# Keeping x by chunks and fetching the first expert's first 128 rows one step earlier, in a fused attention and expert kernel

## What is computed

```python
for t in range(S):                                   # attention
    cur = np.einsum('bhd,bhe->bhde', u[None] * kt, vt)
    y[:, :, t] = np.einsum('bhd,bhde->bhe', rt, state + cur)
    state = w[None, :, :, None] * state + np.einsum('bhd,bhe->bhde', kt, vt)
do_compute = x @ w_skip > 0                          # experts
e_idx = np.argmax(xc @ w_gate, axis=1)
for e in range(E):
    h = np.maximum(xc[mask] @ w1[e], 0.0)
    y[mask] = gate_w[mask, None] * (h @ w2[e])
out[do_compute] = xc + y
h = x @ w_in                                         # dense layer
g = h * np.clip(h + 3.0, 0.0, 6.0) / 6.0
return g @ w_out
```

## Time and profile before

| what | value |
|---|---|
| median of 3 runs | 697.08 us |
| time of the profiled execution | 699.52 us |
| its span in the profile | 697.7 us |
| granted TensorE clock, mean | 0.998 |
| PE, PEld, DVE, ACT, POOL busy | 98, 89, 55, 46, 20 % |
| attention / seam and experts / dense layer | about 0 to 141, 141 to 292, 293 to 697.7 us |

### The profile page before, as it was taken

One profiled execution on the slowest core, in us unless ns is written; L12 is line 12 of the kernel. 1 busy time (PEld: TensorE's weight loads), 2 busy tenths in 40 slices (PEclk: granted clock), 3 DMA queues, 4 the chain that ended last, 5 costly groups with the idle time before them and its releaser, 6 DMA issues.

```text
span 697.7 us, 13712 instructions
## 1 busy us (share of the span) xinstructions
PE 686.7 (98%) x5072; PEld 623.7 (89%) x5072; DVE 381.7 (55%) x788; ACT 323.8 (46%) x704; POOL 141.2 (20%) x190
## 2 busy tenths in 40 slices
PE   7999999999999999999999999999999999999998
PEld 5888888879999999899999999999999989998997
DVE  5677667678777777666543443343434333434333
ACT  5777777735555555554433333233333333324222
POOL 8757966543232321100000000000000000000000
PEclk9999999999999999999999999999999999999999
DMA  7888876718666668320023004000500050001001
GB/s 137 186 201 198 186 170 153 238 39 294 232 216 211 223 208 279 104 25 1 1 60 32 1 1 84 7 1 0 92 1 0 1 91 1 0 1 47 0 1 45
DMA packets 135161, 65.70 MB, mean 94 GB/s; under 512 B 110724, under 2 KB 130696, under 8 KB 135104
## 3 DMA queue, kind: packets, MB, share of 16 engines
q1 hardware_dynamic: 131088, 60.13, 33.6%
q0 software_dynamic: 2560, 4.60, 2.1%
q10 hardware_dynamic: 1456, 0.20, 0.2%
HBM read 53.37 MB, written 12.48 MB: 94 GB/s over the span
## 4 chain that ended last, share of the span: by engine, by line
PE 94%; DVE 2%; POOL 1%; issue 1%; DMA 1%; ACT 0%; another core or an unknown queue 0%; DVEq 0%; ACTq 0%; POOLq 0%
PE bank_A L1038 8%; PE bank_A L1039 8%; PE bank_A L1037 8%; PE bank_L L1037 4%; PE bank_L L1039 4%; PE bank_L L1038 4%; PE bank_P L1039 4%; PE bank_P L1038 4%; PE bank_P L1037 4%; PE bank_kT L1038 4%; PE bank_kT L1039 4%; PE bank_kT L1037 4%; PE bank_A L954 4%; PE bank_YT L1039 3%; PE bank_YT L1038 3%; PE bank_YT L979 3%
## 5 line engine op out<-in xcount | busy, mean ns | idle before, releaser
L1595 DVE TENSOR_TENSOR g_lo<-g,g_hi 128x512 fp32r<-128x512 f32 x96 | 66.5, 692 | 67.1 <-ACT g_hi L824 67.1
L824 ACT ACTIVATE g_hi<-g 128x512 fp32r<-128x512 f32 x96 | 60.7, 632 | 73.1 <-DVE g L1593 73.1
L1593 DVE SCALAR_TENSOR_TENSOR g<-cut,bank_A 128x512 f32<-128x512 f32 x60 | 41.2, 687 | 76.4 <-ACT cut L821 76.4
L821 ACT ACTIVATE cut<-bank_A 128x512 f32<-128x512 f32 x60 | 35.8, 597 | 94.2 <-PE bank_A L1039 93.7
L1039 PE MATMUL bank_A<-mT_hi,wi_lo 128*128 128x512 f32 x180 | 71.0, 394 | 0.0
L1038 PE MATMUL bank_A<-mT_lo,wi_hi 128*128 128x512 f32 x180 | 70.9, 394 | 0.0
L1037 PE MATMUL bank_A<-mT_hi,wi_hi 128*128 128x512 f32 x180 | 70.0, 389 | 0.0
L658 ACT ACTIVATE bank_A<-ident,own 128x128 f32<-128x128 f32 x188 | 58.1, 355 | 23.7 <-DVE A_sb L1293 18.7
L1593 DVE SCALAR_TENSOR_TENSOR g<-cut,bank_kT 128x512 f32<-128x512 f32 x36 | 24.7, 687 | 67.5 <-ACT cut L821 67.5
L821 ACT ACTIVATE cut<-bank_kT 128x512 f32<-128x512 f32 x36 | 21.5, 597 | 70.5 <-PE bank_kT L1039 70.5
L1037 PE MATMUL bank_kT<-mT_hi,wi_hi 128*128 128x512 f32 x108 | 42.1, 389 | 0.9 <-DVE mT_lo L1586 0.9
(11 more groups left out here) (333 smaller groups left out, 1807.1 us busy)
## 6 DMA issues: line engine op xcount, KB each, us to landing
raw<-in_moe_w_dram SPq DMA_DIRECT2D x24, 512.0 KB
raw<-in_moe_w_dram SPq DMA_DIRECT2D x7, 1536.0 KB
r_in<-in_r_dram SPq DMA_DIRECT2D x24, 192.0 KB, 3.6
v_in<-in_v_dram SPq DMA_DIRECT2D x24, 192.0 KB, 4.2
x_scratch<-y_sb SPq DMA_DIRECT2D x24, 192.0 KB, 2.3
k_in<-in_k_dram SPq DMA_DIRECT2D x23, 192.0 KB, 3.8
m_in<-x_scratch SPq DMA_DIRECT2D x20, 192.0 KB, 5.5
out_dram<-o_sb SPq DMA_DIRECT2D x10, 384.0 KB, 2.8
```

Of the source, the lines that this page charges most:

```text
L821: eng.activation(cut[f % 2][:, :], p_H[f % 3][:, :], ACT.Relu, bias=0.5, scale=1.0 / 6.0).then_inc(s_cut, 1)
L824: eng.activation(g_hi[f % 4][:, :], g[f % 2][:, :], ACT.Copy).then_inc(s_ghi, 1)
L1593: eng.scalar_tensor_tensor(g[f % 2][:, :], cut[f % 2][:, :], 1.0, p_H[f % 3][:, :], ALU.min, ALU.mult).then_inc(s_g, 1)
L1595: eng.tensor_tensor(g_lo[f % 4][:, :], g[f % 2][:, :], g_hi[f % 4][:, :].bitcast(F32), ALU.subtract).then_inc(s_glo, 1)
```

## The change

1. x is stored by chunks: row s of chunk c and batch b lies at (c*4 + b)*128 + s. The rows' numbers (`identify`, `own_rows`), the dense layer's blocks (now one chunk of all four batches) and the places of its output rows follow.
2. The first tile's part 0 now holds tokens of chunks 0 to 4 less one, that is 0 to 3. `skip` is worked out one chunk earlier (at b = 1 of chunk 5, for the carry of chunk 4, instead of at b = 2).
3. SP reads the two columns of `listed` by two DMAs: column 0 when chunks 0 to 3 have landed, after the store of (1, 5); column 1 when chunk 4 has landed, between the stores of (2, 5) and (3, 5).
4. POOL gathers part 0 ahead of the scatters of chunk 4, and waits for both columns before the scatters of group 5.
5. PE transposes part 0 right after the last step and puts the two column parts of the first pass around the count of group 6. There are 2 + 2 + 5 + 4 + 8 = 21 `go_on` transposes instead of 5 + 9 + 9 + 8 = 31.
6. ACT's `rows_high(0, 0)` comes ahead of `rows_out(3, 5)`. DVE waits for both columns where it waited for one DMA, and does `rows_low(0, 0)` ahead of `route_slot` of group 6.

```diff
-ON = (8,)
+ON = (2, 5, 4, 8)
         def x_rows(b, c):
-            return x_dram[b * S + c * P:b * S + (c + 1) * P, :]
+            return x_dram[(c * B + b) * P:(c * B + b + 1) * P, :]
@@ SP
-            store(B - 2, NC - 1)
-            for i, done in enumerate(s_slots):
-                eng.wait_ge(done, 16 * B * len(range(i, NC - 1, SETS)))
-            eng.dma_start(listed[:, :, :], slots_by_p[:, 0:TH, :]).then_inc(s_listed, 16)
-            store(B - 1, NC - 1)
+            for t in range(TH):
+                for i, done in enumerate(s_slots):
+                    eng.wait_ge(done, 16 * B * len(range(i, NC - TH + t, SETS)))
+                eng.dma_start(listed[:, t, :], slots_by_p[:, t, :]).then_inc(s_listed, 16)
+                store(B - TH + t, NC - 1)
...
-                    eng.dma_start(out[bass.ds(blk * BLK + half * (BLK // 2), BLK // 2), :].rearrange("(t p) n -> p t n", p=P),
-                                  o_sb[:, ts, :]).then_inc(s_out[half], 16)
+                    eng.dma_start(out_rows[ts, bass.ds(blk * P, P), :].rearrange("b p n -> p b n"), o_sb[:, ts, :]).then_inc(s_out[half], 16)
@@ POOL
-            scatters(NC - 2, NC - 2, range(B))
...
             eng.wait_ge(s_listed, 16)
             for b in range(B):
-                eng.wait_ge(s_st[b], 16 * (NC - b // (B - 1)))
-            rows_of(0, 0, listed, stored=N - P)
+                eng.wait_ge(s_st[b], 16 * (NC - 2))
+            rows_of(0, 0, listed, stored=(NC - 2) * B * P)
+            scatters(NC - 2, NC - 2, range(B))
+            eng.wait_ge(s_listed, 16 * TH)
             scatters(NC - 1, NC - 1, range(0, LATE))
@@ ACT
-            rows_out(B - 1, NC - 1)
-            exponentials(NC, slice(LATE, B))
...
+            rows_high(0, 0)
+            rows_out(B - 1, NC - 1)
+            exponentials(NC, slice(LATE, B))
             eng.wait_ge(s_raw2, 16 * W2_PARTS)
-            for f in range(G1 - 2):
-                w2_high(f)
-            rows_high(0, 0)
-            for f in range(G1 - 2, G1):
+            for f in range(G1):
                 w2_high(f)
@@ PE
+            go_on(2, p_rT)
             half_T(0, 0, 0)
-            go_on(ON[0], p_kT)
+            logits_direct(B - 1)
+            x_transposes(B - 1, NC - 1)
+            for b in range(LATE):
+                own_slots(b)
+            eng.wait_ge(s_gThi, 1)
+            first_half(0, xgT_hi, w1_hi, range(1))
+            go_on(ON[0], p_P)
+            count(NC, p_countB, LATE, B, 1)
             eng.wait_ge(s_rows, NT)
-            eng.wait_ge(s_gThi, 1)
-            first_half(0, xgT_hi, w1_hi)
+            first_half(0, xgT_hi, w1_hi, range(1, 2))
+            go_on(ON[1], p_P)
+            for b in range(LATE, B):
+                m = own_slots(b)
+            m.then_inc(s_own, 1)
+            go_on(ON[2], p_P)
             eng.wait_ge(s_gTlo, 1)
             first_half(0, xgT_lo, w1_hi)
+            go_on(ON[3], p_P)
             first_half(0, xgT_hi, w1_lo, range(1))
             half_T(0, 0, 1)
@@ DVE
-            eng.wait_ge(s_listed, 16)
+            eng.wait_ge(s_listed, 16 * TH)
             eng.tensor_copy(who[0][:, 0, :], listed[:, 0, :])
...
-            route_slot(rts[NC], last, half_B)
...
             rows_low(0, 0)
+            route_slot(rts[NC], last, half_B)
```

More of the change, by code:

```diff
@@ L44 @@
 BT = BLK // P
+assert BT == B and NBLK == NC
 LOG_P = P.bit_length() - 1
@@ L447, in load_m @@
                     eng.dma_start(m_in[o * Q:(o + 1) * Q, :, :].rearrange("i k (a j) -> i k a j", j=Q), squares[o]).then_inc(s_m, 16)
+            out_rows = out.rearrange("(b s) n -> b s n", b=B)
             def blocks(blk, i, first=False, last=False):
@@ L1022, in go_on @@
                     eng.transpose(where[:, 0:P], ident[:, :], ident[:, :])
-            go_on(5, p_rT)
-            logits_direct(B - 1)
-            x_transposes(B - 1, NC - 1)
-            for b in range(LATE):
-                own_slots(b)
-            go_on(9, p_YT)
-            count(NC, p_countB, LATE, B, 1)
-            go_on(9, p_YT)
-            for b in range(LATE, B):
-                m = own_slots(b)
-            m.then_inc(s_own, 1)
             def three(dst, a_hi, a_lo, b_hi, b_lo, start, stop):
@@ L1411, in routing @@
                     eng.wait_ge(s_lt, of + 1)
+                    if c == NC - 1:
+                        eng.tensor_scalar(skip[:, :], p_count[:, B, 0:1], -1.0 / P, 1.0, ALU.mult, ALU.add).then_inc(s_skip, 1)
                     carry(of)
+                    if c == NC - 1:
+                        eng.wait_ge(s_skip, 1)
+                        eng.scalar_tensor_tensor(choice[:, 0, 0:1], skip[:, :], 0.0, choice[:, 0, 0:1], ALU.max, ALU.add).then_inc(s_skip, 1)
+                        eng.wait_ge(s_skip, 2)
                     route_choice(rts[of], p_logit, every)
@@ L1420, in routing @@
                 if b == 2 and c == NC - 1:
-                    eng.tensor_scalar(skip[:, :], p_count[:, B, 0:1], -1.0 / P, 1.0, ALU.mult, ALU.add).then_inc(s_skip, 1)
                     carry(c)
-                    eng.wait_ge(s_skip, 1)
-                    eng.scalar_tensor_tensor(choice[:, 0, 0:1], skip[:, :], 0.0, choice[:, 0, 0:1], ALU.max, ALU.add).then_inc(s_skip, 1)
-                    eng.wait_ge(s_skip, 2)
                     eng.wait_ge(s_direct, LATE)
```

8 lines of the change are left out of this document (4 added, 4 removed).

## The result

The changed kernel took 701.11 us (median of four runs, 700.65 to 702.33), the kernel before 697.17 us beside it (696.63 to 697.37). The ratio is 1.0059, with a 95% interval of 1.0046 to 1.0071: 3.9 us slower. The forecast was 699.9 us, slower. In a second set of runs the same kernel did worse, 705.99 us against 698.47 (ratio 1.0090, 1.0065 to 1.0114), with ten runs between 701.23 and 708.39. So by their times there are two losses: one that every run has, and one of several us that comes in most runs of the second set and in none of the first.

What follows compares the result with a forecast made beforehand. TensorE, with 94% of the chain, was taken to bound the kernel. To the 697.08 us median it added 2.8: 1.0 for the measuring point plus 2.44 for the pause, less 0.6 left to the profiler, giving 699.9 us, range 696.2 to 701.2.

Steps and rivals of the forecast that it cites:

- the likeliest case: Whole kernel: the pause is only in the profiled run, so the change is slower, 699.9 us; chance 0.50.
- column 1: VectorE's new wait before `who<-listed`: column 1 lands at 147.75, VectorE comes at 146.36 and waits 1.4 us.
- the point: Start of the second part's first pass on TensorE, 154.99 us before; claimed to move by +1.0 us, shifting the end equally.
- a pause that the timed runs were to lack: VectorE's 2.40 us wait before `pick`; lacking it, timed runs lose up to 2.44 us more, 0.6 left to the profiler.
- the slack of the next tile: Slot table and next tile's gather come 1.5 us later, TensorE 1.0 later; costs nothing unless a transfer lacked slack, up to +0.5.
- The new one loses 0.85 us.: GpSimd's gather of part 1 falls into VectorE's first `w_lo` and loses 0.85 us waiting for it.
- the block: Part 1's gather held up by `w_lo`: measuring point 156.3 us with it, 155.5 without, so +1.3 or +0.5.
- PE waits some 0.4 us, and the last scores stand behind that wait. It costs nothing here.: TensorE before part 0's transposes: 0.4 us wait from about 141.3, hidden because VectorE is busy with `w_lo` from 142.86.
- the sum from `own_slots` on: TensorE from 149.45: fillers, second pass 1.4 us, eight fillers 1.0, third pass until about 153.5, then part 1.
- The pause explains the whole 2.44 if the timed runs don't have it.: Profiled run stood 2.44 us above the median; the pause before `pick` and the slow clock make some 2.9 us.
- the pause is in every run: Rival on VectorE's pause before `pick`: only +1.0 counts, 698.1 us, range 697.0 to 698.4; chance 0.32.
- This holds unless a transfer had no slack, up to +0.5.: Next tile's slot table and gather, 1.5 us later on GpSimd: no cost, or up to +0.5 us without slack.

Runs made afterwards that it cites:

- e0: The kernel before, unchanged, profiled a second time; its profiled execution took 698.09 us.
- e1: The kernel before with only the storage of x by chunks from the change; ratio 0.9998.
- e18: e16 with chunk 4's scatters split, two ahead of the first gather and two behind it; ratio 1.0048, median 700.06 us.
- e2: The changed kernel with 22 instead of 5 fillers behind the first pass's second column part, in the idle time before `own_slots`; ratio 1.0053.
- e12: The kernel before with SyncE holding the fetch of tile 1's w2 until GpSimd has issued both gathers of that tile; ratio 1.0002.
- e13: The kernel before with GpSimd holding tile 1's second gather until SyncE has issued the w2 fetch; 705.43 us, ratio 1.0094.
- e16: The changed kernel with scores and x transposes ahead of `half_T` on TensorE, and VectorE waiting for column 1 only where it is used; ratio 1.0066.
- e10: The changed kernel with SyncE holding the fetch of tile 1's w2 until GpSimd has issued both gathers of that tile; ratio 1.0093.
- e14: The changed kernel with SyncE holding the fetch of tile 1's w2 until that tile's rows have landed; 705.70 us, ratio 1.0093.
- e17: e16 with part 1's gather ahead of group 5's scatters, and w2 held until tile 1's rows have landed; ratio 1.0113.
- e7: The changed kernel, unchanged, run and profiled again in the second set of runs; 705.99 us, ratio 1.0090.
- e4: The changed kernel with VectorE waiting for column 1 only where it uses it, right before `who`; ratio 1.0088.
- e9: The changed kernel with chunk 4's scatters ahead of the first gather again, and a separate semaphore for column 1; ratio 1.0080.
- e19: The kernel before with GpSimd waiting for chunk 4's second scatter to land before starting the third; ratio 1.0049.
- e3: The changed kernel with 17 instead of 2 fillers behind the last step, in the idle time before part 0's transposes; ratio 1.0074.
- e6: e4 with the scatters of group 5 behind the gather of part 1; ratio 1.0130.

## Why the prediction was right and wrong

*Direction and size.* Slower was the likeliest case, and 701.11 us lies 0.1 inside the range, which ended at 701.2. The mechanism named for it, column 1, is there. But the +2.8 us were 1.0 for the point and 1.8 for a pause that the timed runs were to lack. The runs showed 3.15 for the point against e0, and nothing for the pause, since every trace of the kernel before has it. Two steps failed and largely made up for each other, so that +2.8 came as near to +3.9 as it did is luck. A third step, the slack of the next tile, left out the second loss.

*Right, by its own steps.* The first gather at 138.5 (138.29), the fourth scatter ending near 145 (144.55), the second `listed` issued at 146.25 (145.73), VectorE waiting over 1 us for it (2.02), the gather of part 1 at 151.2 (150.65). The tiles stayed 8, the storage by chunks cost nothing (e1).

*"The new one loses 0.85 us."* It didn't: the gather started 0.07 us ahead of `w_lo` and took 1.01. The scatter at 151.97, which began inside `w_lo`, took 2.00 us and ended 0.89 us behind it. In e18 a scatter that began at 150.52 inside `w_lo` took 2.00 us as well, as the first gather of the earlier trace rows took 1.96. So the delay is there again, and what I missed is that it isn't the gather's own: here it fell on the slot table's next but last scatter. What makes it isn't shown. The sum had taken +1.0 between +0.5 without the block and +1.3 with it, so without the block it would have been 0.5 us lower.

*"PE waits some 0.4 us, and the last scores stand behind that wait. It costs nothing here."* The rows of part 0 came as forecast (transposes at 141.49, forecast 141.7), but TensorE was there at 139.71 instead of 141.3 and waited 1.78 us: without the pause it had nothing to hold it up, and the sum had taken its time from a trace with the pause. In the changed kernel VectorE, without the pause, was through `w_lo` at 141.02 and did stand 1.84 us for these scores. At `pick` it was 2.82 us ahead of e0 (137.35 against 140.17), at `so_far` 0.77 (144.20 against 144.97), at `in_place` 1.35 behind (148.08 against 146.73). The pause had gone, and the two new waits ate it and more.

*The measuring point, +1.0 us.* It was +1.72 us against the profile at hand and +3.15 against e0, where the clock is 1.00 throughout; the spans differ by the same 3.2 us. The step that failed is the sum from `own_slots` on, in which TensorE comes early and waits for part 1: its passes and fillers were reckoned at a clock of 1.00 and ran at 0.50 (from start to start the second pass took 2.7 us and eight fillers 1.6, in e0 1.4 and 0.8), and it came last itself, at 155.47 and without a wait. Part 1's transposes could have begun at about 150.65 + 3.2 = 153.9 us, and the point with 1.24 us more at 155.1. e2 agrees: 155.83, less the 0.68 us that its gather was later, is 155.15. So I estimate the 3.15 us as 1.5 of later rows and 1.6 of clock. The changed kernel has idle stretches of 1.78 and 1.96 us on TensorE where the one before has 1.21 us at most. All 14 timed runs of the changed kernel have a mean granted clock of 0.990 to 0.995, all 75 of the kernel before in the five sets of the experiments 0.995 to 1.000.

*"The pause explains the whole 2.44 if the timed runs don't have it."* Wrong in both halves. It is in all five traces with the order of before (before, e0, e1, e12, e13), and the 2.44 us are 1.43 of slow clock and 1.01 unexplained. The rival "the pause is in every run", 698.1 us, had its premise right and its sum wrong, since it rested on the +1.0. The sum from e0 would have been 697.17 + 3.15 = 700.3 us, against 701.11; the 0.8 us between them stay open. Where the second loss strikes, up to 7 us come on top.

*"This holds unless a transfer had no slack, up to +0.5."* For the second set of runs this step failed worst; in the profile of the first set it held (133.4 behind the point, as before). The rows of tile 1 had 0.1 to 0.6 us to spare against the fetch of w2 in the four traces of before's order (e13 apart). Behind that edge the price is 1.0 us in e16, 1.8 in e10 and 4.5 to 7.3 in the seven others (137.9 to 140.7 against 133.4, e14 and e17 apart). I priced a lateness of 0.5 us as 0.5 us. e13 shows it by making it in the kernel before, where at least 1.7 us of the wait are the order's and not the delay's. Holding the fetch until the rows have landed doesn't mend it (e14).

*Open.* Why the table is later in some runs than the scatters make it. In e7 it was issued 3.0 us behind the last scatter instead of 1.2. The one thing in that gap (DMA queues of e7, 156.5 to 159.6 us, packets, MB, share) is a load of instructions, which falls elsewhere in after:

```profile
q8 instruction: 1, 0.02, 2.7%
```

Such a load also lies in the late stretch of e4, e9, e10 and e18, but not of e19. And in after and e16 one lies between the issue of the table's read and GpSimd's copy of it, which came 3.6 and 3.7 us apart, as in before without a load (3.5). So it is a weak sign and no proof. Nor is it settled which idle stretch brings the clock down: it fell in e12 and e13 at 138.2 us with the point where it always is. And what the first pass and its fillers among the counts cost by themselves was not separated.

## What to carry to other kernels

Before moving work along the list of an engine, look at the orders of issue that the old timing happened to give: where two transfers are issued half a microsecond apart, ask what the second costs behind the first, as that can be several times its lateness (0.8 us behind the fetch cost 1.8 us in e10 and 5.8 in e3). Count the new idle stretches of TensorE twice, once as time and once for the clock behind them, and price what follows at both levels (eight fillers took 1.6 us at 0.50 in the profile after, 0.8 at 1.00 in e0). A pause that no engine explains should be looked for in a second profile of the same kernel before a sum is built on its absence.

## What the hardware showed that I had not expected

- Beside runs of four or five indirect DMAs that GpSimd issued back to back (4.8 to 6.3 us) VectorE got a count 2.4 to 4.1 us late, and in other orders TensorE stood 1.7 to 2.4 us. Both went on 0.8 to 1.1 us behind the end of the run. Runs of two (2.3 and 3.2 us) and three (4.5 us, one of its DMAs 1.89 us long) showed none (e18, e19). But in seven traces of the new order with a run of five (after, e3, e4, e6, e7, e10, e14) no such wait is seen either, and in e3 TensorE had work beside nearly all of that run. So the run is what the pauses stand beside, and what holds the engines up isn't known.
- A gather issued behind 1.5 MB of weights made TensorE wait up to 4.3 us, one that ended 0.1 to 0.6 us ahead of them 0.2 us at most. In e7 the DMA engines carried 372 GB/s in that stretch.
- GpSimd took 0.90 to 0.91 us from its own copy of the ids to the next gather, in all traces.
- A wait for the landing of a scatter of 128 pairs cost GpSimd 3.49 us (e19), where SyncE could issue `listed` 1.2 us behind the last one.
